# A convolution and two feed-forward layers: matmuls of 128 rows against pairs of matmuls of 64 rows

## The reference

```python
def _moe_ref(x, w_in, w_out):
    h = np.maximum(x @ w_in, 0.0)
    return (h * h @ w_out).astype(np.float32)

def _moe2_ref(x, w_in, w_out):
    h = x @ w_in
    g = np.where(h > 0.0, h, np.exp(np.minimum(h, 0.0)) - 1.0)
    return (g @ w_out).astype(np.float32)

def reference(**kwargs):
    ...
    attn_out = _attn_ref(**attn_kwargs)     # the average over 7 positions
    x = attn_out.reshape(B * S, D)
    x = _moe_ref(x=x, **moe_kwargs)
    return _moe2_ref(x=x, **moe2_kwargs)
```

## Time and profile before

| | |
|---|---|
| time, median of 3 runs | 2362.86 us (2362.73 to 2363.0) |
| span of the profiled execution | 2362.3 us |
| PE busy | 2328.2 us (99%), 10,240 matmuls |
| PE weight loads (PEld) | 1925.1 us (81%) |
| DVE busy | 1693.1 us (72%) |
| ACT busy | 1520.5 us (64%) |
| POOL busy | 57.0 us (2%), all at the start |
| DMA | 38.19 MB, mean 16 GB/s |

### The profile page before, as it was taken

One profiled execution on the slowest core, in us unless ns is written; L12 is line 12 of the kernel. 1 busy time (PEld: TensorE's weight loads), 2 busy tenths in 40 slices (PEclk: granted clock), 3 DMA queues, 4 the chain that ended last, 5 costly groups with the idle time before them and its releaser, 6 DMA issues.

```text
span 2362.3 us, 33660 instructions
## 1 busy us (share of the span) xinstructions
PE 2328.2 (99%) x10240; PEld 1925.1 (81%) x10240; DVE 1693.1 (72%) x2807; ACT 1520.5 (64%) x2766; POOL 57.0 (2%) x48
## 2 busy tenths in 40 slices
PE   5999999999999999999999999999999999999999
PEld 3888888888888888888888888888888888888887
DVE  7767777677776677776777767776667777677777
ACT  4766666666666666666666666666666666666664
POOL 6200000000000000000000000000000000000000
PEclk9999999999999999999999999999999999999999
DMA  4000000000000000000000000000000000000000
GB/s 143 19 8 16 9 16 16 9 14 14 12 16 16 7 16 9 16 16 7 16 9 16 16 16 7 16 9 16 16 7 16 9 16 16 7 16 14 12 7 14
DMA packets 66477, 38.19 MB, mean 16 GB/s; under 512 B 1952, under 2 KB 64416, under 8 KB 66464
## 3 DMA queue, kind: packets, MB, share of 16 engines
q1 hardware_dynamic: 66464, 38.03, 5.6%
HBM read 25.44 MB, written 12.58 MB: 16 GB/s over the span
## 4 chain that ended last, share of the span: by engine, by line
PE 97%; DVE 1%; DMA 0%; issue 0%; ACT 0%; SPq 0%; DVEq 0%
PE bank_a L286 10%; PE bank_b L287 10%; PE bank_a L283 10%; PE bank_a L282 10%; PE bank_b L284 10%; PE bank_h L265 10%; PE bank_h L263 10%; PE bank_h L266 10%; PE bank_h L264 10%; PE bank_h L262 10%; DVE conv_b L448 0%; DVE conv_a L448 0%; DVE act_lo L487 0%; DMA raw_down<-in_moe_w_out_dram 0%; DMA x_cols<-in_x_dram 0%
## 5 line engine op out<-in xcount | busy, mean ns | idle before, releaser
L487 DVE TENSOR_TENSOR act_lo<-act,act_hi 128x512 fp32r<-128x512 f32 x1024 | 712.7, 696 | 451.6 <-ACT act L353 448.7
L358 ACT ACTIVATE expo<-bank_h 128x512 f32<-128x512 f32 x512 | 306.5, 599 | 509.6 <-PE bank_h L266 506.3
L342 ACT ACTIVATE relu<-bank_h 128x512 f32<-128x512 f32 x512 | 306.4, 598 | 278.8 <-PE bank_h L266 273.5
L262 PE MATMUL bank_h<-mov_hi_a,up_hi_a 128*128 128x512 f32 x1024 | 399.1, 390 | 20.2 <-DVE mov_lo_b L453 20.2
L286 PE MATMUL bank_a<-act_lo,down 128*128 128x512 f32 x1024 | 399.5, 390 | 9.1 <-DVE act_lo L487 9.0
L263 PE MATMUL bank_h<-mov_lo_a,up_hi_a 128*128 128x512 f32 x1024 | 399.3, 390 | 0.0
L264 PE MATMUL bank_h<-mov_hi_a,up_lo_a 128*128 128x512 f32 x1024 | 399.1, 390 | 0.0
L266 PE MATMUL bank_h<-mov_lo_b,up_b 128*128 128x512 f32 x1024 | 399.1, 390 | 0.0
L265 PE MATMUL bank_h<-mov_hi_b,up_b 128*128 128x512 f32 x1024 | 399.1, 390 | 0.0
L284 PE MATMUL bank_b<-act_hi,down 128*128 128x512 f32 x1024 | 398.8, 389 | 0.0
L282 PE MATMUL bank_a<-act_hi,down 128*128 128x512 f32 x1024 | 398.8, 389 | 0.0
(11 more groups left out here) (45 smaller groups left out, 1861.0 us busy)
## 6 DMA issues: line engine op xcount, KB each, us to landing
x_cols<-in_x_dram SPq DMA_DIRECT2D x32, 536.0 KB, 4.3
out_dram<-res_a SPq DMA_DIRECT2D x32, 256.0 KB, 2.6
raw_up<-in_moe_w_in_dram SPq DMA_DIRECT2D x8, 512.0 KB, 6.3
out_dram<-out_b SPq DMA_DIRECT2D x32, 128.0 KB, 2.3
raw_down<-in_moe_w_out_dram SPq DMA_DIRECT2D x8, 384.0 KB, 7.0
x_cols<-in_x_dram SPq DMA_DIRECT2D x1, 512.0 KB, 4.1
taps<-in_weight_dram SPq DMA_DIRECT2D x1, 7.0 KB, 1.7
```

The source lines that it names most:

```text
L262: pe.matmul(bank, hi, hi_a, start=True, stop=False)
L487: dve.tensor_tensor(act_lo[s][:, :], act32[s][:, :], act_hi[s][:, :].bitcast(F32), ALU.subtract)\
```

## The change

Every matmul now has 64 rows, and they come in pairs: one whose operands lie in partitions 0 to 63 (`LOW`) and one with 64 to 127 (`HIGH`). A pair of steps q is handled at once: step q and step q + 8.

Up-projection: the 192 input channels are three blocks of 64. `mov_a` holds two of them, `mov_b` the third (twice, as before), and the new `mov_s` is `mov_a` with its two halves of partitions exchanged, made by two DMAs of SP (`swap_mov`). The weights are laid out so that partitions 0 to 63 hold those of steps 0 to 7 and 64 to 127 those of steps 8 to 15, three blocks each. The LOW matmuls make the hidden block of step q in one bank, the HIGH matmuls that of step q + 8 in another: 9 products each.

Down-projection: each of the five matmuls of a step is cut in two by rows; LOW adds up in `bank_a[0]`, `bank_b[0]` and HIGH in `bank_a[1]`, `bank_b[1]`. So one set of banks is in use in every half, and at the end of each half the two are added: ACT copies `bank_a[0]` and `bank_b[1]` (`copy_a`, `copy_b`), DVE adds (`add_a`, `add_b`), ACT copies the upper rows of the sum (`copy_b_lo`), and DVE adds those (`add_b_lo`). PE waits for `add_a` before the next half's down-projection touches `bank_a`, and for `add_b` before it touches `bank_b`.

ACT and DVE handle two steps at a time, and PE runs one pair ahead instead of three steps. In the first half DVE's taps are placed two or three to a pair. Loads of the weights are cut by the new layout. In the diff "..." also stands for removed lines; the functions as they were are above.

```diff
+    PAIRS = STEPS // 2
+    R = P // 2
+    CP = PAIRS // CHUNKS
+    LOW, HIGH = slice(0, R), slice(R, P)
+    ROWS = (LOW, HIGH)
...
+        up_hi = [sb(f"up{m}_hi", [P, 3, FF // 2], F32R) for m in (1, 2)]
+        up_lo = [sb(f"up{m}_lo", [P, 3, FF // 2], F32R) for m in (1, 2)]
+        mov_s = [sb(f"mov{h}_s", [P, 2, N], F32R) for h in (0, 1)]
...
-        bank_a = [psum(f"bank_a{h}") for h in (0, 1)]
-        bank_b = [psum(f"bank_b{h}") for h in (0, 1)]
+        bank_a = [psum(f"bank_a{t}") for t in range(2)]
+        bank_b = [psum(f"bank_b{t}") for t in range(2)]
...
+            def swap_mov(half, to):
+                sp.wait_ge(mov_lo_done, 2 * half + 1)
+                for rows, swapped in ((LOW, HIGH), (HIGH, LOW)):
+                    sp.dma_start(mov_s[to][rows, :, :].bitcast(F32), mov_a[to][swapped, :, :].bitcast(F32))\
+                      .then_inc(mov_swapped, 16)
...
+            def up(b, kind, h, q):
+                m, half = kind[h], 2 * b + h
+                if q == 0:
+                    pe.wait_ge(mov_lo_done, 2 * (half + 1))
+                    pe.wait_ge(mov_swapped, 32 * (half + 1))
+                if kind == FIRST and h == 0 and q % CP == 0:
+                    pe.wait_ge(w1_up_done[q // CP], 1)
+                cols = slice(q * P, (q + 1) * P)
+                products = [(mov, i, part, weights) for i, mov in ((0, mov_a), (2, mov_b), (1, mov_s))
+                            for weights, part in ((up_hi, 0), (up_hi, 1), (up_lo, 0))]
+                for n, (mov, i, part, weights) in enumerate(products):
+                    for t, rows in enumerate(ROWS):
+                        done = pe.matmul(bank_h[2 * (q % 2) + t][:, :], weights[m][rows, i, cols],
+                                         mov[h][rows, part, :], start=n == 0, stop=n == len(products) - 1)
+                done.then_inc(h_ready, 1)
+            def down_project(b, kind, h, q):
+                half, before = 2 * b + h, STEPS * (2 * b + h) + 2 * q
+                first, last = q == 0, q == PAIRS - 1
+                used = first and not (kind == FIRST and h == 0)
+                if used:
+                    pe.wait_ge(a_done, half)
+                if kind == FIRST and h == 0 and q % CP == 0:
+                    pe.wait_ge(w1_down_done[q // CP], 2)
+                for t in range(2):
+                    f, s = q + PAIRS * t, 2 * (q % 2) + t
+                    w, hi, start = down[kind[h]], act_hi[s], first and t == 0
+                    pe.wait_ge(hi_ready, before + t + 1)
+                    for cols, begin in ((HI_A, start), (LO_A, False)):
+                        for rows, bank in zip(ROWS, bank_a):
+                            pe.matmul(bank[:, :], w[rows, f, cols], hi[rows, :], start=begin, stop=False)
+                    if used and t == 0:
+                        pe.wait_ge(halves_b_done, half)
+                    for rows, bank in zip(ROWS, bank_b):
+                        pe.matmul(bank[:, :], w[rows, f, HI_LO_B], hi[rows, :], start=start, stop=False)
+                for t in range(2):
+                    f, s = q + PAIRS * t, 2 * (q % 2) + t
+                    w, lo, stop = down[kind[h]], act_lo[s], last and t == 1
+                    pe.wait_ge(lo_ready, before + t + 1)
+                    for cols, banks in ((HI_A, bank_a), (HI_LO_B, bank_b)):
+                        for rows, bank in zip(ROWS, banks):
+                            done = pe.matmul(bank[:, :], w[rows, f, cols], lo[rows, :], start=False, stop=stop)
+                done.then_inc(down_done, 1)
...
             def steps(b, kind):
...
+                for h in range(2):
+                    for q in range(PAIRS):
+                        if q + 1 < PAIRS:
+                            up(b, kind, h, q + 1)
+                        elif h == 0:
+                            up(b, kind, 1, 0)
+                        elif kind != END:
+                            if kind == FIRST:
+                                pe.wait_ge(w2_done, 3 * CHUNKS)
+                            up(b + 1, MIDDLE, 0, 0)
+                        down_project(b, kind, h, q)
+            up(0, FIRST, 0, 0)
...
+            def copy_a(half):
+                act.wait_ge(down_done, PAIRS * (half + 1))
+                act.wait_ge(a_done, half)
+                act.copy(part_a[:, :], bank_a[0][:, :]).then_inc(part_a_done, 1)
+            def copy_b(half):
+                act.wait_ge(halves_b_done, half)
+                act.copy(part_b[:, :], bank_b[1][:, :]).then_inc(part_b_done, 1)
+            def copy_b_lo(half):
+                act.wait_ge(halves_b_done, half + 1)
+                act.wait_ge(b_done, half)
+                act.copy(sum_b_lo[:, :], sum_b[HIGH, :]).then_inc(sum_b_lo_done, 1)
...
+            def elu_pair(b, h, q, between):
+                rounds = elus_before(b, h) + 2 * q
+                act.wait_ge(h_ready, pairs_before(b, h) + q + 1)
+                for t in range(2):
+                    act.activation(expo[t][:, :], bank_h[2 * (q % 2) + t][:, :], ACT.Exp).then_inc(exp_done, 1)
+                reuse(b, h, q)
+                for t in range(2):
+                    s = 2 * (q % 2) + t
+                    act.wait_ge(elu_done, rounds + t + 1)
+                    act.copy(act_hi[s][:, :], act32[s][:, :]).then_inc(hi_ready, 1)
+                    between(t)
...
+                        def between(t):
+                            if kind == FIRST and h == 0:
+                                return
+                            if q == 0 and t == 0:
+                                copy_a(half - 1)
+                            if q == 0 and t == 1:
+                                copy_b(half - 1)
+                            if q == 1 and t == 0:
+                                copy_b_lo(half - 1)
+                        (relu_pair, elu_pair)[kind[h]](b, h, q, between)
...
+            def add_a(half, parity):
+                dve.wait_ge(part_a_done, half + 1)
+                dve.tensor_tensor(sum_a[parity][:, :], bank_a[1][:, :], part_a[:, :], ALU.add).then_inc(a_done, 1)
+            def add_b(half):
+                dve.wait_ge(part_b_done, half + 1)
+                dve.tensor_tensor(sum_b[:, :], bank_b[0][:, :], part_b[:, :], ALU.add).then_inc(halves_b_done, 1)
+            def add_b_lo(half, targets):
+                dve.wait_ge(sum_b_lo_done, half + 1)
                 for target in targets:
...
+                    last = dve.tensor_tensor(target, sum_b[LOW, :], sum_b_lo[:, :], ALU.add)
+                last.then_inc(b_done, 1)
+            def mid_sum(half):
+                add_b_lo(half, (mid_b[LOW, :], mid_b[HIGH, :]))
+            def out_sum(half):
+                add_b_lo(half, (out_b[:, :],))
...
+                if q == 0:
+                    add_a(half, 1 - h)
+                    add_b(half)
+                if q == 1 and (h == 0 or kind == FIRST):
+                    mid_sum(half)
+                if q == 1 and h == 1 and kind != FIRST:
+                    out_sum(half)
...
+                        if kind[h] == 0:
+                            sums(b, kind, h, q)
+                            for t in range(2):
+                                dve.wait_ge(square_done, relus_before(b, h) + 2 * q + t + 1)
+                                lo_part(b, h, q, t)
+                        else:
+                            for t in range(2):
+                                elu(b, h, q, t)
+                            sums(b, kind, h, q)
+                            for t in range(2):
+                                lo_part(b, h, q, t)
```

More of the change, by code:

```diff
@@ L248, in _ @@
+                pool.wait_ge(w2_hi_done, 2 * (c + 1))
+                lo_parts(1, c, w2_done, w2_done, 3 * c)
         @block.tensor
         def _(pe):
[L250 to L266 removed]
@@ L311, in split_w1 @@
             def split_w1(c):
-                cols = slice(c * CF * P, (c + 1) * CF * P)
-                tiles = slice(c * CF, (c + 1) * CF)
-                act.wait_ge(w1_loaded[c], 32)
-                act.copy(up_hi_a[0][:, cols], raw_up[:, 0, cols]).then_inc(w1_hi_done, 1)
-                act.copy(up_b[0][:, cols], raw_up[:, 1, cols]).then_inc(w1_hi_done, 1)
-                act.copy(down[0][:, tiles, 0:D], raw_down[:, tiles, :]).then_inc(w1_hi_done, 1)
+                cols = chunk_cols(c)
@@ new lines, in copy_b, with reuse @@
+            def copy_b(half):
[5 more added lines that the diff above has]
+                act.copy(sum_b_lo[:, :], sum_b[HIGH, :]).then_inc(sum_b_lo_done, 1)
+            def reuse(b, h, q):
+                if not (isinstance(b, int) and b == 0 and h == 0 and q < 2):
+                    act.wait_ge(down_done, pairs_before(b, h) + q - 1)
@@ new lines, in steps @@
+            def steps(b, kind):
+                for h in range(2):
+                    half = 2 * b + h
+                    for q in range(PAIRS):
+                        def between(t):
[8 more added lines that the diff above has]
```

(42 more changed lines are left out.)

345 lines of the change are left out of this document (123 added, 222 removed).

## The result

The changed kernel takes 2282.7 us (median of 4 runs, 2282.45 to 2283.19) against 2362.8 us before: a ratio of 0.966, 95% interval 0.9647 to 0.9674. Forecast were 2271 us; the measured time is 12 us above that and inside the likeliest case's own range (2245 to 2300). The profiled execution has a span of 2280.9 us.

A forecast was written before the change was run, and what follows sets the result against it. PE was taken to bound the kernel by its count of matmul slots: 2204.7 us for pairs + 41.6 ends + 3 first swap + 1.7 last sums + 19 boundaries = 2270.0 span, forecast 2271 us; 8-in-10 range 2225 to 2430.

The forecast's parts named there:

- likeliest case: Whole kernel: the forecast of 2271 us, 3.9% less, own range 2245 to 2300, chance 0.52.
- The count: PE's program: 9728 pairs, 19,456 matmuls, in place of 10,240; 116 us saved at 0.2266 us a pair.
- The length of a pair: PE, steady part: a pair of 64-row matmuls takes one slot, 0.2266 us, high half about 0.11 behind low.
- two reasons given for 0.2266: Pair length: two loads' 0.220 lies just under it; a half streaming alone is no quicker than the whole array.
- The lower bound of 0.220: Weight loads on PE: a pair's two loads, one after the other, take 0.220 us; as pace 2206 us, chance 0.08.
- The rival of added handoffs: PE pairs: each matmul pays 0.013 us beyond its columns in turn, 0.240 a pair, 2401 us; chance 0.21.
- No concurrency: PE's row halves do not run at once: 19,456 full slots, 4455 us; chance 0.13.
- The boundary: End of each second-layer half: PE waits for bank sums and act_lo, 0.6 us for 32 halves, 19 us.
- the walk: Second-layer half's start, ACT and DVE instruction by instruction: bank_b's sum late, stall 0.37; act_lo 0.2 more.
- T + 2.01: T is the end of the previous half's last down pair; DVE's sum of bank_b starts 2.01 us later.
- The upper bound, 1.5 us a half: Boundary stall if each instruction costs its full duration: 48 us in all, 2299 us; chance 0.06.
- The ends: Before the first and after the last matmul: 41.6 us as before, 3 more for mov_s, 1.7 for final sums.

The follow-up runs named there:

- one_more_pair: Changed kernel with one more product in up (low weights by low data of the first block), 20 pairs per pair of steps instead of 19: 2383.15 us.
- groups_of_three: Changed kernel, up-projection only: three matmuls of the low half, then three of the high half, instead of turns: 2282.9 us.
- same_half_in_up: Changed kernel with both matmuls of every up pair in partitions 0 to 63, down keeping pairs in both halves: 3291.2 us.
- copies_first: Changed kernel; in the first pair of steps of a second-layer half ACT copies bank_b right after bank_a, ahead of the second act_hi: 2268.6 us.
- sum_last: Changed kernel; in the second pair of steps of a second-layer half DVE makes the sum into mid_b after both act_lo: 2271.7 us.
- nine_then_nine: Changed kernel, up-projection only: all nine matmuls of the low half, then all nine of the high half: 2557.1 us.

## Why the prediction was right

**The count** was exact: 19,456 matmuls, and a pair is worth a slot (one_more_pair: 100 us net for 512 of them).

**The length of a pair** was right in number, 0.2267 for 0.2266, and wrong in its picture. I had the high half run 0.11 us behind the low one, because loads take turns and start in the program's order. The two loads start 0.003 us apart, as do the two matmuls, and groups_of_three shows that the order of the program does not decide. So of the two reasons given for 0.2266 one holds, that a half which streams by itself needs a slot as the whole array does; the other, that two loads in a row just fit in it, has nothing to do with the result. The lower bound of 0.220 from two loads in a row was thus no bound; the slot of one half alone is what counts. The rival of added handoffs, 2401 us, is out: what a slot has beyond its columns is spent by both halves at once. No concurrency, 4455 us, is out; same_half_in_up shows what two matmuls cost without it at this clock, two slots.

**The boundary** carries the miss. For the first pair of steps the walk was good: the sum of bank_b forecast at T + 2.01 to 2.70, found at 1.96 to 2.65, the stall 0.37 against 0.34. For the second pair the forecast was 0.2 and 0.61 was found; over 30 halves that is 12 us, as much as the whole error. The term that was mis-sized is the work ahead of act_lo: I let the two writes of mid_b and the act_lo behind them follow at 0.60, the spacing behind an act_lo, and they follow at 0.70, each at the end of the one before (1163.20, then act_lo at 1164.62); and ACT's copy of sum_b came 0.65 behind its act_hi, not 0.50. DVE gave the first act_lo at T + 8.36 where I had 8.00, and PE paid it twice, once for each act_lo, with a load exposed each time. The upper bound, 1.5 us a half, held, and the first-layer halves lose nothing, as forecast. copies_first and sum_last take the two stalls away one by one.

The longer spacing could have been read before the change, since the kernel before has these instructions too:

```profile
1131.31 1.37 DVE L474 TENSOR_TENSOR mid_b<-bank_b,res_lo_b 64x512 f32<-64x512 f32 x2
1132.71 0.43 DVE L494 TENSOR_SCALAR expo<-expo 128x512 f32<-128x512 f32 x1
...
1054.70 0.62 ACT L365 CAST act_hi<-act 128x512 fp32r<-128x512 f32 x1
1055.34 0.59 ACT L330 COPY res_lo_b<-bank_b 64x512 f32<-64x512 f32 x1
```

Two writes of mid_b take 1.40 there until the next instruction starts, 0.70 each, and ACT's copy of the upper rows comes 0.64 behind its act_hi. The single write of out_b, in partitions 0 to 63, is followed after 0.60. The slow ones are those that write or read partitions 64 to 127, and the one behind such a write; no run tried whether that is the cause.

**The ends** came to 44 us where 46 were forecast: the first matmul at 23.94 (23.2 forecast), 6.3 us behind the last one's slot (6.7), 14 us of waits and lower clock in the first tile (16). The list of waits has one for mov_s, the first, so the later swaps cost nothing, as forecast. The median lies 1.8 us above the span and not 0.5.

The sum against the profiled execution: 2205 for the pairs, 44 for the ends, 29 for the halves in the loop, 2 for the last two halves, 2280 of 2280.9.

## What to carry to other kernels

Count slots: when PE is dense, a change to its program is worth the slots that it saves and no more, here 512 of 10,240, and three blocks of 64 rows fit better in pairs of half arrays than in full ones. Keep one height of matmul throughout a loop, since every change costs about a slot. And when more sums must be read at a boundary, walk ACT and DVE instruction by instruction with the spacing that the trace has for just that instruction: the order in which they serve the boundary and the next step was worth 29 us here, over a third of the change's gain (the other 4 of the 33 us are the earlier start).

## What the runs showed of the hardware

- With all matmuls in partitions 0 to 63, PE stayed for 8.3 ms without a pause at the lengths of the lower clock (0.427 a slot, 0.625 a record). With 18 of 28 slots in one half and the other ten in both, it was at the upper level in the whole steady part (0.2267 a slot). I had expected the upper level in the first and left it open in the second. Why the first stayed low was not tried further.
- A change between 64-row and 128-row matmuls costs 0.24 us in the steady part with two in a pair of steps and 0.22 with four; by the whole times it is 0.204 net (1024 of them 208.6 us, 2048 of them 416.5), because the longer pair of steps hides the boundary stalls. Of it 0.11 is a load that does not start under the matmul before it, as it otherwise does.
- The two row halves take their matmuls separately and out of the program's order: past two of the other half's without loss, past three in nine_then_nine, but not past four (0.54 us lost per pair of steps).
- Two loads of 64 rows run at once, 0.003 us apart. They are as long as a load of 128 rows: 0.184 against 0.188.
- Two matmuls in one half take two slots at the upper clock (same_half_in_up), two in different halves one.
